# The last half tile of keys on 128 rows: one product with V instead of two, and turns that are 64 columns wide

## The reference

```python
scores = scale * np.matmul(q_rot, k_rot.transpose(0, 1, 3, 2))
scores = scores - np.max(scores, axis=-1, keepdims=True)
attn = np.exp(scores)
attn = attn / (np.sum(attn, axis=-1, keepdims=True) + 1e-09)
x = np.matmul(attn, v)                      # then (batch, 576, 512)
u = x + (x.transpose(0, 2, 1) @ U @ V).transpose(0, 2, 1)
out = u + np.maximum(u @ w_ch1, 0.0) @ w_ch2
```

## Time and profile before

| | us |
|---|---|
| runs, median of 3 | 799.39 (798.22 to 800.57) |
| profiled execution | 799.79 |
| its span | 797.7 |
| first scores on TensorE | 22.3 |
| plain stretch, heads without mixing steps | 48 to 114 |
| last products with V end | 365.2 |
| stage B on TensorE | 390.4 to the end |

### The profile page before, as it was taken

One profiled execution on the slowest core, in us unless ns is written; L12 is line 12 of the kernel. 1 busy time (PEld: TensorE's weight loads), 2 busy tenths in 40 slices (PEclk: granted clock), 3 DMA queues, 4 the chain that ended last, 5 costly groups with the idle time before them and its releaser, 6 DMA issues.

```text
span 797.7 us, 11651 instructions
## 1 busy us (share of the span) xinstructions
PE 725.8 (91%) x4336; PEld 655.4 (82%) x4336; DVE 373.0 (47%) x619; ACT 373.4 (47%) x807; POOL 260.1 (33%) x182
## 2 busy tenths in 40 slices
PE   0799998989898989987499999999999999999998
PEld 0689887778787878775499999999999999999997
DVE  2689897788778897786411121121212112122112
ACT  1689998789878989774433211111210111111100
POOL 6667758556866658300455200000000000000000
PEclk9999999999999999999799999999999999999999
DMA  7856665577457753523763030011003003001001
GB/s 239 237 147 188 174 189 139 152 225 197 127 164 227 205 164 90 130 70 119 219 243 128 1 119 1 0 61 59 1 1 118 1 1 119 0 1 40 1 1 39
DMA packets 45942, 86.47 MB, mean 108 GB/s; under 512 B 7552, under 2 KB 20032, under 8 KB 43840
## 3 DMA queue, kind: packets, MB, share of 16 engines
q1 hardware_dynamic: 45456, 84.50, 35.9%
q10 hardware_dynamic: 432, 1.25, 0.4%
HBM read 43.25 MB, written 14.16 MB: 72 GB/s over the span
## 4 chain that ended last, share of the span: by engine, by line
PE 50%; DVE 1%; ACT 0%; issue 0%; DVEq 0%
PE ps L842 25%; PE ps L855 25%; DVE utl L802 1%; DVE res L809 0%; ACT wh L777 0%; DVE wl L813 0%; DVEq L808 0%
## 5 line engine op out<-in xcount | busy, mean ns | idle before, releaser
L819 DVE SCALAR_TENSOR_TENSOR htl<-ps,hth 128x384 fp32r<-128x384 f32 x96 | 53.5, 558 | 325.8 <-ACT hth L794 325.8
L794 ACT ACTIVATE hth<-ps 128x384 fp32r<-128x384 f32 x96 | 47.2, 492 | 328.1 <-PE ps L842 328.1
L496 DVE TENSOR_REDUCE negmax<-ps 128x1 f32<-128x576 f32 (+1 forms) x160 | 120.2, 751 | 55.1 <-PE ps L602 53.7
L602 PE MATMUL ps<-stack 128*128 128x288 f32 (+1 forms) x640 | 125.3, 319 | 22.3 <-DMA stack<-raw 22.3
L842 PE MATMUL ps<-uth,wh 128*128 128x384 f32 x384 | 130.1, 339 | 10.1 <-DVE utl L802 10.1
L412 ACT ACTIVATE prob<-ps,negmax 128x576 f32<-128x576 f32 (+1 forms) x160 | 118.4, 740 | 41.8 <-DVE negmax L496 40.9
L842 PE MATMUL ps<-uth,wl 128*128 128x384 f32 x384 | 130.0, 338 | 0.0
L842 PE MATMUL ps<-utl,wh 128*128 128x384 f32 x384 | 129.5, 337 | 0.0
L502 DVE TENSOR_TENSOR ptl<-ps,pth 128x512 fp32r<-128x512 f32 (+1 forms) x192 | 121.4, 646 | 3.6 <-ACT pth L421 1.9
L855 PE MATMUL ps<-wl,hth 128*128 128x512 f32 x288 | 114.0, 396 | 0.0
L620 PE MATMUL ps<-ident,prob 128*128 128x128 f32 (+1 forms) x672 | 97.7, 270 | 17.7 <-ACT prob L412 16.1
(11 more groups left out here) (65 smaller groups left out, 860.4 us busy)
## 6 DMA issues: line engine op xcount, KB each, us to landing
stack<-raw SPq DMA_DIRECT2D x192, 144.0 KB, 2.6
raw<-in_qk SPq DMA_DIRECT2D x16, 1152.0 KB, 5.5
tables<-in_w SPq DMA_DIRECT2D x11, 512.0 KB, 4.5
raw<-scratch_ut SPq DMA_DIRECT2D x6, 768.0 KB, 6.7
res<-scratch_u SPq DMA_DIRECT2D x18, 256.0 KB, 3.5
out<-res SPq DMA_DIRECT2D x18, 256.0 KB, 2.1
vraw<-in_v SPq DMA_DIRECT2D x16, 256.0 KB, 5.3
scratch_u<-xn SPq DMA_DIRECT2D x16, 256.0 KB, 3.2
```

The source lines that it names most:

```text
L496: nc.vector.tensor_reduce(negmax[0:w, n % NT:n % NT + 1], scores_of(n, w), AX.XY, ALU.max, negate=True).then_inc(maxed, 1)
L602: mm = nc.tensor.matmul(ps[0:w, at_:at_ + CH], stack[:, r % 2, i, 0, P * t:P * t + w], stack[:, r % 2, i, part, CH * c:CH * c + CH], start ...
L794: nc.scalar.activation(hth[:, i % 2], up_bank(i), ACT.Relu).then_inc(relu_hi, 1)
L819: nc.vector.scalar_tensor_tensor(htl[:, i % 2], up_bank(i), 0.0, hth[:, i % 2], ALU.max, ALU.subtract).then_inc(relu_lo, 1)
```

## The change

It has three parts.

**Both parts of the half tile on 128 rows.** The fifth key tile's lo part goes into rows 64 to 127 of `pth`, below its hi part, and `ptl` keeps four tiles. V's half tile stands twice in the 128 rows of its place, so one product of 128 rows gives hi times V plus lo times V. Each group has nine products. For TAIL VectorE writes 64 rows of 512 columns to `pth[64:128]`. For LAST it needs two operations, one of four tiles by 64 columns into `ptl` and one of 64 x 64 into `pth[64:128]`. `pt_lo` now counts 7 per head (`lows_done`), and the bank of LAST is free after both.

**Turns of 64 columns.** TAIL's source is `prob[:, ..., 512:576]`, and its result has 64 rows. ScalarE rounds 64 rows of it.

**Loading.** V comes in one DMA of all 128 rows. The clearing of V's buffers is gone, and with it SyncE's wait at the start.

```diff
@@ _release
-        eng.wait_ge(e["pt_lo"], UNITS * i + rest[0] + 1)
+        eng.wait_ge(e["pt_lo"], lows_done(i, rest[0]))
+def lows_done(g, j):
+    return LOWS * g + j + 1 + (1 if j >= LAST else 0)
...
@@ load
-                sp.dma_start(vraw[:, r % 2, 0:NT - 1], v[r][:, 0:NT - 1]).then_inc(v_loaded[r % 2], 16)
-                sp.dma_start(vraw[0:WT[-1], r % 2, NT - 1], v[r][0:WT[-1], NT - 1]).then_inc(v_loaded[r % 2], 16)
+                sp.dma_start(vraw[:, r % 2], v[r]).then_inc(v_loaded[r % 2], 16)
...
-            sp.wait_ge(zeroed, 2)
             load(0)
...
-            cleared = [vraw[:, 0], vraw[:, 1], prob[:, :, S:SP_], xh[D:P, NT - 1].bitcast(F32),
+            cleared = [prob[:, :, S:SP_], xh[D:P, NT - 1].bitcast(F32),
...
@@ round_p
-                nc.scalar.activation(pth[:, g % 2, keys, queries], source, ACT.Copy).then_inc(pt_hi, 1)
+                rows = slice(0, D if j == TAIL else P)
+                nc.scalar.activation(pth[rows, g % 2, keys, queries], source, ACT.Copy).then_inc(pt_hi, 1)
...
@@ split_p
-                nc.vector.tensor_tensor(ptl[:, g % 2, keys, queries], source, pth[:, g % 2, keys, queries],
-                                        ALU.subtract).then_inc(pt_lo, 1)
+                if j != TAIL:
+                    full = slice(0, NT - 1)
+                    nc.vector.tensor_tensor(ptl[:, g % 2, :, queries], source[:, full], pth[:, g % 2, full, queries],
+                                            ALU.subtract).then_inc(pt_lo, 1)
+                if j >= LAST:
+                    mine = source[0:D, source.shape[1] - 1:source.shape[1]]
+                    nc.vector.tensor_tensor(pth[D:P, g % 2, NT - 1:NT, queries], mine,
+                                            pth[0:D, g % 2, NT - 1:NT, queries], ALU.subtract).then_inc(pt_lo, 1)
...
@@ times_v
-                products = [(kt, part) for kt in range(NT) for part in (pth, ptl)]
+                products = [(kt, part) for kt in range(NT - 1) for part in (pth, ptl)] + [(NT - 1, pth)]
...
-                    pe.wait_ge(pt_lo, UNITS * g + (TAIL + 1 if second else -(-CH // P)))
+                    pe.wait_ge(pt_lo, lows_done(g, TAIL if second else CH // P))
...
@@ transposes
-                                                 prob[:, (NT * g + t) % NP, P * (NT - 1):SP_], ident[:, :])
+                                                 prob[:, (NT * g + t) % NP, P * (NT - 1):S], ident[:, :])
...
+    vp[:, S:] = vp[:, P * (NT - 1):S]
```

## The result

| | before | after |
|---|---|---|
| median of the runs, us | 798.85 (4 runs, 798.22 to 800.57) | 803.18 (4 runs, 802.67 to 803.97) |
| ratio to before | | 1.0040, 95% interval 1.0027 to 1.0053 |
| profiled execution / span | 799.79 / 797.7 | 803.61 / 801.7 |
| mean granted clock | 0.987 | 0.983 |

The change makes the kernel slower by 0.4%. The forecast was 799.9 us, no change. The median of 803.18 lies 0.4 us above the upper end of the range, 802.8. The two medians of four runs stand 0.54% apart; by the ratio, 1.0040 on 799.39, the time would be 802.6, just inside. Either way the change costs several times the +0.5 us of the sum.

A forecast was written before the change was run, and what follows sets the result against it. ScalarE nearly full in plain heads, TensorE leading in mixing stretches: plain heads +0.4, batches +0.3, first heads 0, last head -0.1, start -0.1 sum to +0.5 us, giving 799.9 us (no change), range 796.8 to 802.8.

The forecast's parts named there:

- What bounds the kernel: Attention stage: ScalarE nearly without holes in plain heads; TensorE leads in mixing stretches, where latency around waits decides.
- the product: Product groups with V: one product in ten goes, 0.13 us for each of 64 groups, ceiling 8.3 us of TensorE.
- the change of rows: VectorE's splits: 0.11 to 0.12 us lost at each change of rows written, before the first new operation and the following maximum.
- Plain heads: Heads without mixing work: +0.05 and +0.06 us through one pair, 7 heads x 0.055 = +0.4 us.
- The margin of a few hundredths: Plain heads: ScalarE's exponential at 69.26 would be left with 0.04 us of slack.
- rival C: Plain heads: VectorE takes TensorE's place, +0.15 us per head x 31 = +4.6, 804.0 us; chance 0.17.
- 5 to 8: TensorE's busy time over the kernel: expected to fall by 5 to 8 us.
- VectorE's pair +0.28 stands in front of the long preparation there, then a group at half clock gives -0.24: 0: First two heads: the later VectorE pair and the shorter half-clock group were taken to cancel, 0 us.
- -0.24: Groups at half clock, products 0.24 us apart: one product less gives -0.24 us, in the first heads and once per batch.
- the clock's 1.1 us at most: Any forecast: a stretch at half clock comes or goes, at most 1.1 us for ten products.
- -0.1, bounds 0 and -1.4: Start: SyncE no longer waits 1.4 us for V's clears, but the same bytes end at the same time, -0.1 us.
- The turns of 64 columns: Last half tile's transposes: nothing taken; a rival had them 50 ns faster, -1.5 us, 798.4 us, chance 0.06.

The follow-up runs named there:

- b_nine: Kernel before with nine products per group, the fifth key tile's lo part by V left out, nothing else changed: 794.95 us, ratio 0.9936.
- a_ten: Kernel after with a tenth product again in each group (fourth key tile's lo part taken twice), VectorE's two operations kept: 807.28 us, ratio 1.0088.
- a_norow: Kernel after with the half tile's lo part written to rows 0 to 63 of a spare buffer instead of rows 64 to 127: 797.02 us, ratio 0.9960.
- a_spread: Kernel after with VectorE's two 32-row splits of the mixing constants moved one and two pairs of slots later: 799.61 us, ratio 0.9995.
- a_flip: Kernel after with the fifth key tile's halves swapped, read from row 64, lo part written from row 0, turns of 128 columns: 804.61 us, ratio 1.0058.
- a_start: Kernel after with the old start: GpSimd clears both V buffers, SyncE waits for that before its first load: 802.76 us, ratio 1.0039.
- a_ident: Kernel after with the identity on its own semaphore, so VectorE and GpSimd no longer wait for it: 803.85 us, ratio 1.0047.
- c_best: Kernel before with the new loading, the identity's own semaphore, and the three mixing-constant splits on GpSimd in slots 15, 25, 35: 796.87 us, ratio 0.9960.

## Why the prediction was right in its core and wrong in its time

- **What bounds the kernel; the product; the change of rows: right.** 0.12 to 0.13 us per head of a plain pair for the product (b_nine, a_ten), 0.11 to 0.12 on VectorE per change of rows (a_norow), distances within 0.01 us. From the 2nd to the 8th landmark ScalarE stands still for 2.55 us before and 2.58 after, as forecast; in the fixed window of 66 us it is 2.2 and 3.0, because the heads lie elsewhere in it. Plain heads +0.07 per pair, forecast +0.11; 29 heads with three batches +0.3, forecast about +0.7. The margin of a few hundredths held, and rival C did not come, although the time that it gave, 804.0, is near the result. Its number would have been right for a wrong reason: a_ten tells them apart. One sign failed: TensorE is busy 3.4 us less and not 5 to 8, and why is open; the longer low clock lengthens its work, but in six plain heads, with the clock up, it is also only 0.36 us less, where 12 products at 0.13 make 1.6.
- **"VectorE's pair +0.28 stands in front of the long preparation there, then a group at half clock gives -0.24: 0": the step that failed.** It moved the preparation by 0.28 and asked only what comes behind it on VectorE, not what runs beside it. Counted from the first landmark, the preparation did come 0.30 us later, and GpSimd's split of V 0.08 earlier. GpSimd's split of V started 0.2 us behind the second 32-row operation, and its 1.97 us against 1.56 in all later heads was the sign, in the trace of before, that the two can't run together. That shift changed which of them waits: +1.2 us on the path that sets the first head. a_norow, with the shift taken back, turns the order round again, and a_spread, without the pair, has GpSimd's split at 1.54 us. The Trainium skill, SBUF — State Buffer, section Who interferes with whom, has this: a VectorE instruction with two inputs from SBUF contends with a GpSimd one that reads SBUF, the port that they share is an exclusive lock, and the order of issue decides which of them blocks. The trace agrees: GpSimd ran from 38.28 to 39.86, and VectorE's operation, started at 38.5, ended at 40.47. That is 0.61 behind GpSimd's end, where it takes 0.75 alone, so 0.14 us of it still ran beside the other.
- **"-0.24" of the half clock, and the clock's 1.1 us at most: under-sized.** The first head took 12.2 to 12.4 us where GpSimd waited (before, b_nine, a_norow), with the clock low for 3.4 us. Where VectorE waited it took 12.36 with no fall of the clock (a_ten), 13.6 to 13.8 with 3.4 us of low clock (a_flip, a_start), and 14.6 to 14.8 with 6.8 us (after, a_ident). At the same length of low clock, then, the wait is worth 1.2 to 1.5 us, and the low clock costs up to 2.4. In the batches the -0.24 was counted three times, and the trace of before has two such stretches there (212 to 216 and 301 to 304 us).
- **The start, "-0.1, bounds 0 and -1.4": wrong sign.** I took the tables as first in the queue and the bytes as the same. The earlier load of q and k shares the DMA engines with the tables from 0.74 us on, and the second pair comes in at 7.59, ahead of the end of the tables: +0.45 at the first scores. That it comes from the second pair is argued, not shown.
- **The turns of 64 columns: nothing seen, not settled.** No run changed them alone. With 128 columns a_flip's pair is 0.09 longer, which its third loss of 0.12 explains as well.
- **The 1.0 us at stage B: the clock, and whether the change brings it is open.** TensorE's hole ahead of it is the same (9.64 and 9.67 us), but the clock was low from 382.9 to 393.2 us before and from 385.3 to 399.0 after:

```profile
390.00:394.00 4.00, 3.20 (x10) 2.86 (x11) 3.83 (x4) 1.63 (x2) 3.35 (x2) 0.60 0.39 133
```

```profile
394.00:398.00 4.00, 3.72 (x12) 3.21 (x11) 2.82 (x2) 1.06 (x1) 4.00 (x2) 0.50 0.46 160
```

The longer stretch is not tied to the change alone: c_best, built on the kernel before, takes 408.4 us from the first product of stage B to the end, and a_ten, built on the kernel after, 407.3. But eight of the nine traces built on the kernel after have it, and one of the five built on the one before. Among runs of one kernel the span moves with the clock: 53 runs of the kernel before have spans of 798.4 us (median of 20) at a mean clock of 0.985, 797.0 (28) at 0.987 and 796.4 (5) at 0.989. The four of after are 800.7 and 800.8 at 0.985, 801.7 and 802.0 at 0.983. At the same mean clock, 0.985, the change costs 2.4 us, 0.3%. That is the start (0.45), VectorE's wait in the first head (1.2 and the 0.3 that brought it about) and the heads (0.3), together 2.3; this attribution is a sum of separate readings, and no run shows the 2.4 by itself. The runs of after at 0.983 lie another 1.1 us higher, as the two lengths of the low clock in the first head do (a_start and after, 13.78 and 14.62).

## What to carry to other kernels

When an edit shifts an engine's stream by some tenths, look at what runs beside it on the engine that shares a resource with it: an operation of unusual length in the trace (1.97 among 1.56) marks a pair that already excludes each other, and the one on the path may be the next to wait. An operation that reads or writes from row 64 among operations that start at row 0 costs the overlap with its neighbours twice, here 0.23 us of VectorE's time and 0.13 us of a head; that is what one product with V gives, so stacking the two parts on 128 rows gained nothing. A wait that holds back a load can be what gives another load its share of the DMA engines; taking it away is a change of order, not a gain.

## What the hardware showed that I had not expected

- Two VectorE operations of 0.75 us took 2.76 us beside one of GpSimd, against 1.53 with the order of the starts reversed, and GpSimd then 1.97 to 2.11 instead of 1.56. The five traces in which VectorE started later and the three in which GpSimd did agree.
- VectorE's loss of overlap follows the row at which inputs start, not the output's alone (a_flip).
- With SyncE's first load issued at 0.74 us and not at 2.08, the table of sines, issued at the same time as before (1.15 and 1.18 us), took 8.6 us to land and not 4.3, and VectorE's first operation started 0.46 us later.
- The span of one kernel differs by 1.1 to 1.4 us between groups of runs whose mean clocks differ by 0.002 (0.985 and 0.987 before, 0.983 and 0.985 after), which is more than this change's whole effect in the heads.
